# Attention in 32 head pairs: q and k of two heads transposed side by side, stacked by SBUF copies, q_hi by k_lo on 64 partitions

## The reference

```python
scores = scale * np.matmul(q, k.transpose(0, 1, 3, 2))
thresh = np.max(scores, axis=-1, keepdims=True) - tau
scores = np.where(scores >= thresh, scores, -1000000000.0)
scores = scores - np.max(scores, axis=-1, keepdims=True)
attn = np.exp(scores)
attn = attn / (np.sum(attn, axis=-1, keepdims=True) + 1e-09)
return np.matmul(attn, v).astype(np.float32)
```

## Time and profile before

| what | value |
|---|---|
| median of 3 runs | 1362.42 us |
| the profiled execution | 1362.08 us, span 1360.3 us |
| PE busy | 1325.3 us (97%) |
| PEld busy | 1161.0 us (85%) |
| DVE busy | 893.7 us (66%) |
| ACT busy | 876.1 us (64%) |
| POOL busy | 322.5 us (24%) |
| mean granted TensorE clock | 0.990 of full speed |

### The profile page before, as it was taken

How to read it: one execution, slowest core, us unless ns; L and a number is a source line. 1 busy time by engine, 2 the same in 40 slices (tenths; PEclk the granted TensorE clock), 3 DMA queues, 4 the chain that set the end, 5 groups by cost and what they waited for, 6 DMA issues and landing times.

```text
span 1360.3 us, 30705 instructions
## 1 busy us (share of the span) xinstructions
PE 1325.3 (97%) x9628; PEld 1161.0 (85%) x9628; DVE 893.7 (66%) x1969; ACT 876.1 (64%) x2086; POOL 322.5 (24%) x433
## 2 busy tenths in 40 slices
PE   6999999999999999996999999999999999999998
PEld 5777777777777777774999999999999999999997
DVE  4777777777777777775766765576647665756544
ACT  5888888888888888884545544554445445534432
POOL 3455554455544555533000000000000000000000
PEclk8999999999999999997999999999999999999999
DMA  8534433334333344322010011001110111011000
GB/s 234 131 101 113 116 94 105 104 103 116 101 103 104 99 115 116 93 77 87 19 34 17 18 34 42 19 18 34 34 40 5 34 34 34 1 42 34 17 9 32
DMA packets 141082, 90.49 MB, mean 67 GB/s; under 512 B 96192, under 2 KB 125120, under 8 KB 140992
## 3 DMA queue, kind: packets, MB, share of 16 engines
q1 hardware_dynamic: 137360, 82.47, 21.6%
q10 hardware_dynamic: 3632, 6.88, 1.5%
HBM read 70.29 MB, written 25.31 MB: 70 GB/s over the span
## 4 chain that ended last, share of the span: by engine, by line
PE 52%; DVE 1%; ACT 0%; issue 0%; DVEq 0%
PE kv_ps L805 15%; PE kv_ps L886 15%; PE vr_ps L805 15%; PE y_ps L870 7%; DVE mixed L998 0%; DVE xm_lo L1004 0%; ACT mixed L918 0%; DVE x L1057 0%; ACT xm_hi L926 0%; ACT y L935 0%; DVE square L1015 0%; DVE g_lo L1030 0%; DVE x_lo L1062 0%; DVE gated L1025 0%; ACT g_hi L966 0%
## 5 line engine op out<-in xcount | busy, mean ns | idle before, releaser
L566 DVE SCALAR_TENSOR_TENSOR probs<-score_ps,threshold,probs 128x576 f32<-128x576 f32 x288 | 234.5, 816 | 72.2 <-ACT probs L506 70.4
L561 DVE TENSOR_REDUCE neg_max<-score_ps 128x1 f32<-128x576 f32 x288 | 209.8, 747 | 95.6 <-PE score_ps L434 93.3
L506 ACT ACTIVATE probs<-score_ps,neg_max 128x576 f32<-128x576 f32 x288 | 215.3, 747 | 0.0
L487 ACT ACTIVATE probsT<-aux_ps 128x512 f32<-128x512 f32 x288 | 168.2, 615 | 44.3 <-PE aux_ps L395 44.3
L395 PE MATMUL aux_ps<-ident,probs 128*128 128x128 f32 x1280 | 190.5, 279 | 3.9 <-ACT k_raw L487 2.6
L434 PE MATMUL score_ps<-k_lo,qT 128*128 128x288 f32 x512 | 166.5, 340 | 5.0 <-DVE probs L566 4.2
L805 PE MATMUL kv_ps<-xm_hi,w_lo 128*128 128x288 f32 x512 | 152.5, 298 | 13.9 <-DVE xm_lo L1004 11.1
L395 PEld LDWEIGHTS aux_ps<-ident,probs 128*128 128x128 f32 x1280 | 144.5, 141 | 24.8 <-ACT probsT L487 10.9
L805 PE MATMUL kv_ps<-xm_hi,w_hi 128*128 128x288 f32 x512 | 152.5, 298 | 0.0
L805 PE MATMUL kv_ps<-xm_lo,w_hi 128*128 128x288 f32 x512 | 152.3, 297 | 0.0
L886 PE MATMUL kv_ps<-kk_hi,w_hi 128*128 128x288 f32 x512 | 151.1, 295 | 0.0
(11 more groups left out here) (99 smaller groups left out, 3216.7 us busy)
## 6 DMA issues: line engine op xcount, KB each, us to landing
k_nat<-in_k SPq DMA_DIRECT2D x128, 128.0 KB, 2.5
recip_rows<-recip_scratch SPq DMA_DIRECT2D x64, 144.0 KB, 3.1
x_scratch<-x_out SPq DMA_DIRECT2D x32, 288.0 KB, 2.6
out<-y SPq DMA_DIRECT2D x36, 256.0 KB, 2.0
q_nat<-in_q SPq DMA_DIRECT2D x31, 256.0 KB, 2.8
v_nat<-in_v SPq DMA_DIRECT2D x31, 256.0 KB, 2.7
w_stage<-packed SPq DMA_DIRECT2D x32, 192.0 KB, 2.5
x_in<-x_scratch SPq DMA_DIRECT2D x8, 578.0 KB, 4.1
```

The lines of the kernel that those rows point to most:

```text
L487: return nc.scalar.activation(out, in_, ACT.Copy)
L506: nc.scalar.activation(tile_halves(i), scored(i), ACT.Exp, bias=neg_max[:, i:i + 1], scale=1.0).then_inc(exp_done, 1)
L561: nc.vector.tensor_reduce(neg_max[:, i:i + 1], scored(i), mybir.AxisListType.XY, ALU.max, negate=True).then_inc(max_ready, 1)
L566: nc.vector.scalar_tensor_tensor(tile_halves(i), scored(i), threshold[:, i:i + 1], tile_halves(i), ALU.is_ge, ALU.mult, accum_out=row_sum[ ...
```

## The change

q and k are loaded with the two heads of a pair side by side (qk_nat: 64 columns of head 0, 64 of head 1; the last 64 positions of q and k in rem_nat), k only once. One transposed tile then has head 0 on partitions 0 to 63 and head 1 on 64 to 127. So there is one step k0, one q0 and one kq0 with a single transpose; k1 and q1 are gone, and the plans are written anew. Both q and k are split behind the transpose by GpSimd (q_all and q_lo; k_hi and k_lo); q_all has room for two copies. SP then copies between the halves of the partitions, eight copies within SBUF per pair: stack_q puts q_lo beside q_hi (q_all) and q_hi onto the other half (q_swap), stack_k puts k_hi onto both halves and parts of k_lo onto the other half (k_swap). The first pair's k is split by VectorE, as before.

A score tile is, for each half of the keys, one full matmul of q_all (hi and lo) with k_hi, and one of q_hi with k_lo that uses 64 partitions: half 0 on partitions 0 to 63, half 1 on 64 to 127, next to each other in the order and into different banks. The product q_lo by k_lo is left out. scores0 waits for q_stacked and k_stacked.

In SP's run(c), stack_q(c+1) stands behind the loads of q and k, stack_k(c+1) behind load_v(c+1). On GpSimd split_q(c+1) and split_k(c+1) come ahead of split_w. The diff, cut ("..." marks what is left out):

```diff
 PE_PLAN = steps("""
-    scores0 probs3- probs7- scores1 pv0- scores2 probs6- probs8- scores3 q0 rem1- scores4
-    probs0 pv1- kq0 scores5 k0 rem0 scores6 probs2 k1 scores7 probs1 q1 scores8 probs4 probs5
+    probs1- scores0 q0 probs7- scores1 probs6- pv0- scores2 kq0 probs8- scores3 probs0 scores4
+    rem1- k0 scores5 pv1- scores6 probs2 probs4 scores7 probs5 rem0 scores8 probs3
 """)
 ACT_PLAN = steps("""
-    probs3- exp8- probs7- exp0 exp1 pv0- probs6- probs8- q0 rem1- probs0 exp2 exp3 exp4 pv1-
-    kq0 k0 rem0 exp5 probs2 k1 exp6 probs1 q1 exp7 probs4 probs5
+    probs1- q0 probs7- exp8- probs6- exp0 exp1 pv0- kq0 probs8- exp2 probs0 rem1- k0 exp3 exp4
+    exp5 pv1- probs2 probs4 exp6 probs5 rem0 exp7 probs3
 """)
 DVE_PLAN = steps("""
-    max8- max0 max1 mask8- mask0 mask1 recip0- max2 max4 max3 mask2 mask3 max5 mask4 max6
-    mask5 max7 mask6 mask7
+    max0 max1 mask8- mask0 mask1 max2 recip0- max3 mask2 max4 max5 mask3 mask4 mask5 max6 max7
+    mask6 mask7 max8
 """)
-FIRST_PREPARE = steps("k0 kq0 k1 q0 q1")
+FIRST_PREPARE = steps("k0 kq0 q0")
...
+    QW = KW = S + REM
+    H1 = QW + REM
...
-        q_nat = sb("q_nat", [P, 2, TILES, D])
-        k_nat = sb("k_nat", [P, 2, TILES, 2, D])
+        qk_nat = sb("qk_nat", [P, 2, 2, FULL, 2 * D])
+        rem_nat = sb("rem_nat", [P, 2, 2 * D])
         v_nat = sb("v_nat", [P, 2, TILES, D])
-        q_split = sb("q_split", [P, TILES, 2, D])
-        qT = sb("qT", [P, 2, 2, MAIN], F32R)
-        q_rem = sb("q_rem", [P, 2, 4, REM], F32R)
-        k_raw = sb("k_raw", [P, 2 * S])
-        k_hi = sb("k_hi", [P, 2, 2 * S + REM], F32R)
-        k_lo = sb("k_lo", [P, 2, 2 * S + REM], F32R)
+        q_raw = sb("q_raw", [P, QW])
+        k_raw = sb("k_raw", [P, KW])
+        q_lo = sb("q_lo", [P, QW], F32R)
+        q_all = sb("q_all", [P, 2, 2 * QW + REM], F32R)
+        q_swap = sb("q_swap", [P, 2, QW + REM], F32R)
+        k_hi = sb("k_hi", [P, 2, S + KW], F32R)
+        k_lo = sb("k_lo", [P, 2, KW], F32R)
+        k_swap = sb("k_swap", [P, 2, HALF + REM], F32R)
...
+        def load_qk(eng, n, name, it, c, loaded):
+            for h in range(2):
+                eng.dma_start(qk_nat[:, c % 2, n, :, h * D:(h + 1) * D],
+                              heads[name][it * 4 + (2 * c + h), 0:MAIN, :].rearrange(
+                                  "(p t) d -> p t d", t=FULL)).then_inc(loaded[c % 2], 16)
+            eng.dma_start(rem_nat[n * REM:(n + 1) * REM, c % 2, :].rearrange("p (h d) -> p h d", h=2),
+                          heads[name][bass.ds(it * 4 + 2 * c, 2), MAIN:S, :].rearrange(
+                              "h p d -> p h d")).then_inc(loaded[c % 2], 16)
         def load_q(eng, it, c):
-            load(eng, q_nat[:, c % 2, :, :], "q", it, c, q_loaded[c % 2])
+            load_qk(eng, 0, "q", it, c, q_loaded)
+        def load_k(eng, it, c):
+            load_qk(eng, 1, "k", it, c, k_loaded)
...
-                def load_k(it, c):
-                    slot = c % 2
-                    for twice in range(2):
-                        for h in range(2):
-                            head = it * 4 + (2 * c + h)
-                            k_to = k_nat[:, slot, :, twice, :]
-                            sp.dma_start(k_to[:, h * FULL:(h + 1) * FULL, :], heads["k"][head, 0:MAIN, :].rearrange(
-                                "(p t) d -> p t d", t=FULL)).then_inc(k_loaded[slot], 16)
-                            sp.dma_start(k_to[REM * h:REM * (h + 1), MIX, :],
-                                         heads["k"][head, MAIN:S, :]).then_inc(k_loaded[slot], 16)
+                def stack_q(it, c):
+                    par = c % 2
+                    sp.wait_ge(q_steps, count(it, c, 3, 2))
+                    sp.dma_start(q_swap[REM:P, par, 0:QW].bitcast(F32), q_all[0:REM, par, 0:QW].bitcast(F32)).then_inc(q_stacked, 16)
+                    sp.dma_start(q_swap[0:REM, par, REM:].bitcast(F32), q_all[REM:P, par, H1:].bitcast(F32)).then_inc(q_stacked, 16)
+                    sp.wait_ge(q_steps, count(it, c, 3, 3))
+                    sp.dma_start(q_all[REM:P, par, 0:QW].bitcast(F32), q_lo[0:REM, :].bitcast(F32)).then_inc(q_stacked, 16)
+                    sp.dma_start(q_all[0:REM, par, H1:].bitcast(F32), q_lo[REM:P, :].bitcast(F32)).then_inc(q_stacked, 16)
+                def stack_k(it, c):
+                    par = c % 2
+                    sp.wait_ge(k_steps, count(it, c, 3, 3))
+                    sp.dma_start(k_hi[REM:P, par, 0:S].bitcast(F32), k_hi[0:REM, par, 0:S].bitcast(F32)).then_inc(k_stacked, 16)
+                    sp.dma_start(k_hi[0:REM, par, S:].bitcast(F32), k_hi[REM:P, par, S:].bitcast(F32)).then_inc(k_stacked, 16)
+                    sp.dma_start(k_swap[0:REM, par, :].bitcast(F32), k_lo[REM:P, par, 0:HALF + REM].bitcast(F32)).then_inc(k_stacked, 16)
+                    sp.dma_start(k_swap[REM:P, par, 0:HALF].bitcast(F32), k_lo[0:REM, par, REM + HALF:].bitcast(F32)).then_inc(k_stacked, 16)
...
                         load_q(sp, it, c + 2)
-                        load_k(it, c + 2)
+                        load_k(sp, it, c + 2)
                     if c < PAIRS - 1:
+                        stack_q(it, c + 1)
                         if c > 0:
                             sp.wait_ge(aux_full, turns(it, number_of(c - 1, "pv", 1) + 1))
                         load_v(sp, it, c + 1)
+                        stack_k(it, c + 1)
...
-                load_k(0, 0)
+                load_k(sp, 0, 0)
                 load_q(sp, 0, 1)
-                load_k(0, 1)
+                load_k(sp, 0, 1)
+                stack_k(0, 0)
+                stack_q(0, 0)
...
-                def split_q(it, c):
-                    wait(q_loaded[c % 2], count_loaded(it, c, 3))
-                    nc.gpsimd.tensor_copy(q_split[:, :, 0, :].bitcast(F32R), q_nat[:, c % 2, :, :]).then_inc(q_steps, 1)
-                    wait(q_steps, count(it, c, 2, 1))
-                    nc.gpsimd.tensor_tensor(q_split[:, :, 1, :], q_nat[:, c % 2, :, :], q_split[:, :, 0, :],
+                def split_q(it, c, run):
+                    wait(aux_copied, turns(it, 1 + max(number(run, (x, 0, False)) for x in ("q", "kq"))))
+                    for at in (0, H1):
+                        nc.gpsimd.tensor_copy(q_all[:, c % 2, at:at + QW], q_raw[:]).then_inc(q_steps, 1)
+                    wait(q_steps, count(it, c, 3, 1))
+                    nc.gpsimd.tensor_tensor(q_lo[:], q_raw[:], q_all[:, c % 2, 0:QW].bitcast(F32),
                                             ALU.subtract).then_inc(q_steps, 1)
                 def split_k(it, c, run):
-                    for h in range(2):
-                        ready = max(number(run, ("k", h, False)), number(run, ("kq", 0, False)))
-                        wait(aux_copied, turns(it, ready + 1))
-                        to = slice(h * S, (h + 1) * S)
-                        hi, lo = k_hi[:, c % 2, :], k_lo[:, c % 2, :]
-                        if h == 1:
-                            nc.gpsimd.tensor_copy(hi[:, 2 * S:], k_raw[:, S:S + REM])
-                        nc.gpsimd.tensor_copy(hi[:, to], k_raw[:, to]).then_inc(k_steps, 1)
-                        wait(k_steps, count(it, c, 4, 2 * h + 1))
-                        if h == 1:
-                            nc.gpsimd.tensor_tensor(lo[:, 2 * S:], k_raw[:, S:S + REM], hi[:, 2 * S:].bitcast(F32),
-                                                    ALU.subtract)
-                        nc.gpsimd.tensor_tensor(lo[:, to], k_raw[:, to], hi[:, to].bitcast(F32),
-                                                ALU.subtract).then_inc(k_steps, 1)
+                    wait(aux_copied, turns(it, 1 + max(number(run, (x, 0, False)) for x in ("k", "kq"))))
+                    nc.gpsimd.tensor_copy(k_hi[:, c % 2, S:], k_raw[:]).then_inc(k_steps, 1)
+                    nc.gpsimd.tensor_copy(k_hi[:, c % 2, 0:S], k_raw[:, REM:]).then_inc(k_steps, 1)
+                    wait(k_steps, count(it, c, 3, 1))
+                    nc.gpsimd.tensor_tensor(k_lo[:, c % 2, :], k_raw[:], k_hi[:, c % 2, S:].bitcast(F32),
+                                            ALU.subtract).then_inc(k_steps, 1)
...
                         sums(it, c - 1)
-                        split_w(it, c - 1)
                     if c < PAIRS - 1:
+                        split_q(it, c + 1, c)
                         split_k(it, c + 1, c)
                     if c > 0:
+                        split_w(it, c - 1)
                         normalize(it, c - 1)
-                    if c < PAIRS - 2:
-                        wait(aux_full, turns(it, prepared(c)))
-                        split_q(it, c + 2)
...
+                def query(qq, h, i, par, base):
+                    at = base[h] + (0 if i == MIX else (2 + h) * REM + i // 2 * P)
+                    return qq[:, par, at:at + P]
...
-                                pe.wait_ge(aux_copied, turns(it, prepared(c - 1)))
-                                pe.wait_ge(k_steps, count(it, c, 4, 2))
```

(80 more changed lines are left out.)

24 lines of the change are left out of this document (9 added, 15 removed).

## The result

The changed kernel takes 1674.99 us (median of 4 runs, 1672.10 to 1676.82), before 1362.11 in the same series: 1.2295 times as long, 95% interval 1.2273 to 1.2316. The profiled execution took 1675.37 us, its span is 1673.5.

The account below looks back on a forecast made before the run. SP's queue of DMA issues behind its wait for recip_T was to bound each pair: 9.75 + 0.3 + 16.85 = 26.9 us, 8.28 more than now; with pair 30 and the start +248.5, so 1611 us, range 1540 to 1680.

Parts of the forecast that it names:

- SP's chain: SP's queue per pair, from spread's first issue through loads and stacking to the last copy's landing: 16.85 us.
- The stretch from scores0 to recip_T: Attention pair, from scores0 to spread's first issue: 8.43 us today, +1.3 by ScalarE's new order, so 9.75.
- The clock: TensorE restarting each pair at half clock after idling some 8 us: +0.3 us per pair, bounds 0 and 1.9.
- the two parts of the pair: Scores0 to spread's first issue, 9.75 + 0.3 us forecast; from there to the next scores0, 16.85 forecast.
- The rival with 1.6 us more (1659): TensorE's restart at low clock costs its upper bound, 1.6 us more in 30 pairs: 1659 us; chance 0.20.
- The start: Before the attention's first scores: splits, stacking and more issues ahead of the small loads cost +4 us, an estimate.
- The row tiles: 64-partition score matmuls on TensorE: -0.13 us run together, +0.3 for mode switches, so a tile 0.17 us dearer.
- Together cost one slot: Score tiles on TensorE: two 64-partition matmuls run together take one matmul's slot, -0.13 us.
- one after the other: Score tiles on TensorE: the two 64-row matmuls do not run together, +20 us, 1631; chance 0.13.
- no relief: Stacking hidden, but TensorE is the bound and mode switches eat the savings: +12 us, 1374; chance 0.04.
- faster: Stacking on SP hidden, only lighter engines count: ScalarE's 1.24 us per pair saved, 1324 us; chance 0.03.
- the signs named: Profile after: recip_T every 27 us, TensorE waiting 7 to 9 us for copies, low clock, 64-row matmuls starting together.

Follow-up runs that it names:

- Loads first: Changed kernel with SP's six loads of q and k moved ahead of its wait for recip_T: 1524.91 us (one run).
- the reorder: Changed kernel, SP's loads and stack_q ahead of the recip_T wait, stack_k between spread's halves, load_v last: median 1364.3 us, 1.0021 times before.
- the filler: Changed kernel with 32 useless ident matmuls on TensorE ahead of its wait for the copies: 1615.47 us (with 64: 1804.69).
- full matmuls with the copies hidden: Changed kernel with SP's issues reordered and all scores by 128-row matmuls, k_lo stacked like k_hi: 1332.68 us, 0.9796 times before.

## Why the prediction was right, and where it was off

- The range was 1540 to 1680, and 1675 lies 5 us inside its upper end: the path was right, and one of its terms was far off. (The lower bound given as 1539 comes to 1541 by the sum; nothing hangs on it.)
- SP's chain: 16.85 us forecast from the first issue of spread to the landing, 16.8 to 17.2 measured. In part that is luck, for in the pair shown the issues took 0.9 us more than their terms (six loads 0.3, stack_q 0.3, the rest of the chain 0.2), and the landing and the waits set apart took 0.6 less. The copies are issued 0.57 to 0.65 us apart (440.55, 441.14; 445.16 to 447.07 for three), taken at 0.6; the last lands after 2.1 us, taken at 2.7; the six loads took 440.55 - 436.14 = 4.41, taken at 4.10. Loads first and the reorder show that this chain, and not the copies' traffic, is the loss: both keep all eight copies.
- The stretch from scores0 to recip_T, without the clock: 9.75 forecast, 9.93 with the filler.
- The clock is the term that was mis-sized: +0.3, "bounds 0 and 1.9", against 2.1 us, above its own upper bound. It makes 29 times 1.8, about 52 of the 64 us between 1611 and 1675; most of the rest is some 0.2 us each in the two parts of the pair. The rival with 1.6 us more (1659) was the truer case. I let ScalarE's waits of before swallow TensorE's slower first steps. But after an idle time there is no backlog: ScalarE waits for the very first transposes, q0's four transposes begin 1.32 us after scores0 in place of 0.77 with the filler (449.39 to 450.71, 366.56 to 367.33), and take 1.11 in place of 0.66 us. ScalarE's first copy is then 1.0 us later in these two pairs (2.47 against 1.46 behind scores0), and the copy of pv0 2.5 us (8.14 against 5.62), which is all that recip_T loses: the whole delay is there once pv0 is done.
- The start: +4 forecast for what stands before the first scores, and scores0 of pair 0 did come 4.6 us later (18.64 against 14.01). But the first recip_T came 11.4 us later: the rest of pair 0 took 3.6 us more, and the first part of pair 1 3.1. The end of the attention gave 3.9 back.
- The row tiles: forecast -0.13 us for two at once and +0.3 for the switches, +0.17 per tile. Measured +0.22, but of other parts. Two pairs behind one another are 0.24 us apart, where two full matmuls take 0.26: the pair saves only 0.02. The switches then take the rest, 0.24, inside the bounds of nothing and 0.36 and near the 0.3 taken. The row behind that 0.3 was misread, though: in the trace of before the four 64-column transposes start in two pairs 0.107 us apart (340.265 and 340.372), so that they take 0.21 us and not "at most as much" as one full transpose, and the switches there cost some 0.14 and not 0.25 to 0.36. That 0.3 came out so near for 64 rows is luck. "Together cost one slot" failed; the rival "one after the other" is wrong in the mechanism (both start at one time) and nearly right in the price, which in the changed kernel showed only ahead of recip_T.
- The Trainium skill says that changing the tiling mode drains TensorE ("TensorEngine Tiling (Array Packing)", Key Properties). The 0.24 us that the switches cost here fit that; the rows do not show what the time goes into. Its "Up to 2×" for a dimension of at most 64 (the same page, Theoretical Speedup) does not appear in these rows: two 64-row matmuls at once are 1.1 times as fast as two full ones (0.24 against 0.26 us).
- The rival "no relief" (the copies hidden, TensorE giving the savings back) is what the reorder turned out to be: 1364 against the 1374 worked out. The rival "faster" (1324) is what full matmuls with the copies hidden come near to: 1333. Both needed the second part under 8.9 us, and it is about 7 there.
- The Trainium skill says that the sequencer's time to initiate a DMA "is usually small relative to the DMA itself" ("DMA: Bandwidth & Descriptors", Issuing engines are not separate DMA queues). Here one issue takes 0.6 us and its landing 2.1 to 3.1, but 21 issues stand behind one wait, and their sum decides: six of them moved past the wait changed the time by 150 us.
- Of the signs named, TensorE's waits for k_swap (8.1 us each), the low clock and the two row tiles starting together came true; a pair takes 29 and not 27 us, and SP waits 12.3 us for recip_T where 9 to 10 from scores0 were expected, mostly by the clock.

## What to carry to other kernels

Before adding a DMA to a queue that seems idle, write down what that queue waits for and count every issue between that wait and the new one (0.6 us each here): prefetches that cost nothing where they stood become the critical path once something urgent stands behind them. Put urgent issues in front of patient ones, and a wait that comes late behind both. When a change makes TensorE idle in every turn of a loop (here 3.4 or 8 us), price its restart at half clock: after 8 us it was granted 0.50 for the next 4.6 us, and 2.1 us were lost until recip_T. Set no slack of the busy state against it.

## What the runs showed that I had not expected

- TensorE's granted clock was 0.58 on average in the idle stretch from 444.0 to 449.4, 0.50 in the 4.6 us after work began again and 0.92 over the next 7. That half clock costs 2.1 us in a pair of 29, and filling the gap with 7.3 us of useless matmuls took 60 us off the kernel. An idle stretch of 3.4 us was enough for much of it: with the loads first the first part is 11.5 us, against 9.9 with the filler.
- A float32 matmul of 128 columns that is no transpose was two instructions and 0.23 us (32 of them: x64 and 7.31 us in the row); a transpose of the same size is one, and follows the one before after 0.11.
- Two row tiles of 64 partitions start within 0.01 us of each other, but the next two come 0.24 us later for 288 columns, while a full matmul follows every 0.13 us. So at this size two 64-row matmuls at once gain next to nothing over two full ones (0.02 us); why (their weight loads, or the two banks they write) was not tested.
